# Soft mixture of experts after a causal attention and an MLP on one core: the slot weighting of three of four batches moved into the last MLP

## What is computed

```python
# 1 attention with a causal mask and a decay from the running sum of log f
scores = q @ k.T / 8 + (cum_i - cum_j)          # masked above the diagonal
x = softmax(scores) @ v                         # to (2304, 512)
# 2 MLP
h = x @ w_in                                    # (2304, 2048)
x = (h * sigmoid(1.702 * h)) @ w_out            # (2304, 512)
# 3 soft mixture of experts: 8 experts, 4 slots each = 32 slots
logits = x @ phi                                # (2304, 32)
d = exp(logits - logits.max(0)); d /= d.sum(0) + 1e-9      # over all tokens
slot_input = d.T @ x                            # (32, 512), 4 rows per expert
slot_out[e] = relu(slot_input[e] @ w1[e]) @ w2[e]          # 512 -> 1024 -> 512
c = exp(logits - logits.max(1)); c /= c.sum(1) + 1e-9      # over the slots
result = c @ slot_out                           # (2304, 512)
```

## Time and profile before

| | us |
|---|---|
| median of three runs | 764.37 (763.54 to 765.16) |
| the profiled execution, its own time | 765.94 |
| its span, first to last instruction | 764.2 |
| mean granted clock of TensorE | 0.983 of full |
| PE busy | 717.7 (94% of the span) |
| DVE / ACT / POOL busy | 444.7 / 437.0 / 399.3 |
| chain that ended last | PE 79%, DVE 10%, ACT 7%, issue 2% |

### The profile page before, as it was taken

How to read it: one execution, slowest core, us unless ns; L and a number is a source line. 1 busy time by engine, 2 the same in 40 slices (tenths; PEclk the granted TensorE clock), 3 DMA queues, 4 the chain that set the end, 5 groups by cost and what they waited for, 6 DMA issues and landing times.

```text
span 764.2 us, 15776 instructions
## 1 busy us (share of the span) xinstructions
PE 717.7 (94%) x6027; PEld 681.0 (89%) x6027; DVE 444.7 (58%) x1255; ACT 437.0 (57%) x1031; POOL 399.3 (52%) x439
## 2 busy tenths in 40 slices
PE   3999979999999999999999999999999999998993
PEld 3888879999999999999999989999999999995562
DVE  5898957676776646675656466766542332224323
ACT  4788866575757675666576665757554344311113
POOL 4355357474747764565657564848385476520000
PEclk9999989999999999999999999999999999998897
DMA  4433323332333333333331413332214454598976
GB/s 104 106 92 106 94 65 89 87 94 81 95 94 96 95 94 81 87 105 91 100 91 51 126 28 95 94 108 67 69 43 141 135 169 163 161 401 348 357 307 247
DMA packets 90362, 96.65 MB, mean 126 GB/s; under 512 B 61296, under 2 KB 61296, under 8 KB 88240
## 3 DMA queue, kind: packets, MB, share of 16 engines
q1 hardware_dynamic: 90288, 95.66, 40.6%
HBM read 90.84 MB, written 4.79 MB: 125 GB/s over the span
## 4 chain that ended last, share of the span: by engine, by line
PE 79%; DVE 10%; ACT 7%; issue 2%; DMA 0%; POOL 0%; SPq 0%; DVEq 0%; POOLq 0%
PE mb L1204 51%; PE yb L1057 6%; PE zb L1076 6%; PE xb L1103 5%; PE mb L1256 2%; DVE prob L838 2%; PE xb L1037 2%; ACT prob L689 2%; PE yb L1295 1%; ACT xh L713 1%; DVE ptl L844 1%; PE yb L1059 1%; DVE kl L806 1%; DVE qs L802 1%; ACT qs L681 1%
## 5 line engine op out<-in xcount | busy, mean ns | idle before, releaser
L1204 PE MATMUL mb<-xh,wih 128*128 128x288 f32 x512 | 159.1, 311 | 7.8 <-DVE xl L855 4.3
L1204 PE MATMUL mb<-gh,woh 128*128 128x288 f32 x512 | 156.5, 306 | 3.5 <-DVE x2t L932 3.5
L1204 PE MATMUL mb<-xl,wih 128*128 128x288 f32 x512 | 151.6, 296 | 0.0
L1204 PE MATMUL mb<-xh,wil 128*128 128x288 f32 x512 | 151.6, 296 | 0.0
L1204 PE MATMUL mb<-gl,woh 128*128 128x288 f32 x512 | 150.8, 294 | 0.0
L1204 PE MATMUL mb<-gh,wol 128*128 128x288 f32 x512 | 150.8, 294 | 0.0
L643 POOL TENSOR_TENSOR gl<-hid,gh 128x288 fp32r<-128x288 f32 x128 | 105.0, 825 | 74.9 <-ACT gh L730 73.3
L925 DVE SCALAR_TENSOR_TENSOR hid<-gate,mb 128x288 f32<-128x288 f32 x128 | 57.7, 451 | 116.0 <-ACT gate L736 114.9
L689 ACT ACTIVATE prob<-prob,m_row 64x576 f32<-64x576 f32 (+4 forms) x160 | 96.4, 604 | 35.3 <-DVE m_row L824 34.4
L660 POOL TENSOR_TENSOR wol<-stage,woh 128x512 fp32r<-128x512 f32 x64 | 82.9, 1295 | 62.0 <-ACT woh L675 62.0
L660 POOL TENSOR_TENSOR wil<-stage,wih 128x512 fp32r<-128x512 f32 x64 | 82.1, 1290 | 57.0 <-ACT wih L675 56.9
(11 more groups left out here) (196 smaller groups left out, 1471.1 us busy)
## 6 DMA issues: line engine op xcount, KB each, us to landing
stage<-in_moe_w_in SPq DMA_DIRECT2D x64, 256.0 KB, 3.0
stage<-in_moe_w_out SPq DMA_DIRECT2D x64, 256.0 KB, 2.6
ring_a<-in_moe_w SPq DMA_DIRECT2D x16, 1024.0 KB, 6.9
ring_b<-in_moe_w SPq DMA_DIRECT2D x14, 1024.0 KB, 11.8
cum_b<-cum_dram SPq DMA_DIRECT2D x32, 288.0 KB, 3.7
qk_in<-in_q SPq DMA_DIRECT2D x32, 144.0 KB, 3.0
qk_in<-in_k SPq DMA_DIRECT2D x32, 144.0 KB, 3.5
v_in<-in_v SPq DMA_DIRECT2D x32, 128.0 KB, 3.2
```

The costliest lines, as they stand in the source:

```text
L1204: ins = mm(bank[:, 0:HALF], a[:, t, P * (j % 4):P * (j % 4) + P], x[:, t, cols], start=(i == 0), stop=(i == 11))
```

## The change

Steps of kind `early` are put into the list of the last MLP. On the data of batches 0 to 2 (15 tiles) they make the maximum per slot, the weights `ew`, their exp, their sum (`all_sum`) and the 15 weighting products, kept unscaled in `acc`. Batch 3 is weighted after the last unit with its own maximum per row of its slot-major logits (`bmax`, `low_max`), without turning the logits first, by exp with a sum on ACT (`et`), a turn of the result (`ewt`), and 5 weighting products. `kept` rescales `acc`, and the factor between the row's maximum and that of all four column groups (`factor`), with the reciprocal of the sum, goes into the selecting matrix `sel_f`. The turned logits of batch 3, needed for c alone, are made after the experts' input. `post 1` turns the first two of four column tiles of tokens 256 to 575 before unit 63; `post 2` does the rest, with the slot logits of the first three of four tiles of the contraction ahead of the wait for unit 63's eviction. The ring has 11 places: `ring_x` becomes two, loaded in units 33 to 47; `ring_a` is loaded in quarters at each odd unit up to 31; matrices 0 to 5 are loaded inside the MLP. The constant products are 4, 2, 8 and 5 where they were 9, 3 and 14. The tile memory is laid out anew to fit. Two memsets of `mb` and `yb` (L970, L971) go. In the diff below the removed lines of the joint (L941 to L973, L1212 to L1246) and declarations are left out, and from the loads on twelve leading spaces of each line.

```diff
 LAST_POST = ((0, 1), (2, 3, 4))
+AHEAD = 2
...
-TURN_AT = 6
+TURN_AT = 7
 SOFTMAX_AT = (8, 9, 10, 11, 18, 19, 20, 21)
 SOFTMAX_EXP = 13
-BUSY = (9, 3, 14)
+BUSY = (4, 2, 8, 5)
+EARLY = 3 * QT
+EARLY_AT = {"maxima": 10, "turn_max": 12, "max": 13, "spread": 15, "weigh": 16, "exp": 17, "sums": 19,
+            "send0": 20, "send1": 21, "send2": 22, "send3": 23, "total": 24, "keep": 26}
+RING_X_AT = 33
...
+        if m == BATCH - 1:
+            steps += [(0, ("early", kind)) for kind in EARLY_AT if EARLY_AT[kind] == u]
...
-    return (held_steps(m) + mlp_steps(m, 0, U_MLP - 2) + [(0, ("post", 0))]
-            + mlp_steps(m, U_MLP - 2, U_MLP) + [(0, ("post", 1))])
+    return (held_steps(m) + mlp_steps(m, 0, U_MLP - 2) + [(0, ("post", 0))] + mlp_steps(m, U_MLP - 2, U_MLP - 1)
+            + [(0, ("post", 1))] + mlp_steps(m, U_MLP - 1, U_MLP) + [(0, ("post", 2))])
...
-        ring = ring_a + ring_b + [ring_x[:, :]]
+        ring = ring_a + ring_x + ring_b
...
-        if last and j == 2:
+        if last and u % 2 and u // 8 < len(ring_a):
             sp.wait_ge(x_lo, 4 * BATCH)
-            load_half_expert(u // 16, u % 16 // 8)
+            load_expert_part(u // 8, u // 2 % 4, 4)
+        at = u - RING_X_AT
+        if last and at >= 0 and at % 2 == 0 and at // 8 < len(ring_x):
+            sp.wait_ge(acc_made, 1)
+            load_expert_part(len(ring_a) + at // 8, at // 2 % 4, 4)
...
         sp.wait_ge(unit_done, m * U_MLP + U_MLP - 8)
-        load_expert(4)
-        load_expert(5)
+        load_expert(6)
+        load_expert(7)
...
-        load_expert(6)
+        load_expert(8)
...
+        load_expert(9)
+        load_expert(10)
...
+    elif st == ("early", "exp"):
+        act.wait_ge(ew_sub, 1)
+        nc.scalar.activation(ew[:, :, :], ew[:, :, :], ACT.Exp).then_inc(ew_exp, 1)
...
+    elif st == ("post", 1):
+        for i in LAST_POST[1]:
+            act.wait_ge(post_token, m * QT + i + 1)
+            nc.scalar.copy(x2last[0:QW[i], i, 0:P * AHEAD], last_tokens[i][0:QW[i], 0:P * AHEAD]
+                           ).then_inc(ahead_out, 1)
+    elif st == ("post", 2):
+        act.wait_ge(max_made, 2)
+        nc.scalar.activation(et[:, :], last_logits[:, 0:P + 64], ACT.Exp, bias=low_max[:, 1:2],
+                             accum_out=bsum[:, :]).then_inc(e_made, 1)
+        nc.scalar.activation(kept[:, :], low_max[:, 0:1], ACT.Exp, scale=-1.0, bias=low_max[:, 1:2]
+                             ).then_inc(kept_made, 1)
+        act.wait_ge(post_token, m * QT + QT + 2)
+        nc.scalar.copy(x2last[:, 2, P * AHEAD:MODEL], last_tokens[2][:, P * AHEAD:MODEL]).then_inc(token_out, 1)
...
-nc.scalar.activation(ew[:, :, :], ew[:, :, :], ACT.Exp).then_inc(t_act, 1)
+nc.scalar.copy(x2last[:, 3, P * AHEAD:MODEL], last_tokens[3][:, P * AHEAD:MODEL]).then_inc(token_out, 1)
+act.wait_ge(top_spread, 1)
+act.wait_ge(top_made, 1)
+nc.scalar.activation(factor[:, :], top_back[:, 0:1], ACT.Exp, bias=top[:, 0:1]).then_inc(factor_made, 1)
+nc.scalar.copy(lt[0:SLOTS, P:P + 64], last_logits[0:SLOTS, P:P + 64])
+nc.scalar.copy(lt[:, 0:P], last_logits[:, 0:P]).then_inc(lt_last, 1)
...
+        early(st[1])
+    elif st == ("post", 0):
+        nc.vector.memset(last_logits[32:64, P:P + 64], -3e38)
+        nc.vector.memset(last_logits[64:P, P:P + 64], -3e38).then_inc(edge_made, 1)
+    elif st == ("post", 2):
         dve.wait_ge(post_logits, m + 2)
-        keep_turned(last_logits)
-        dve.wait_ge(lt_turned, m + 1)
-        keep_logits(last_turn)
-        keep_maxima(m)
-        keep_values(m)
+        nc.vector.tensor_reduce(bmax[:, :], last_logits[:, 0:P + 64], AX_X, ALU.max).then_inc(max_raw, 1)
+        dve.wait_ge(max_raw, 1)
+        nc.vector.tensor_scalar(low_max[:, 1:2], bmax[:, :], -1.0, low_max[:, 0:1], ALU.mult, ALU.min
+                                ).then_inc(max_made, 1)
     elif st[0] == "unit":
         unit(b, m, st[1])
+def early(kind):
+    if kind == "maxima":
+        for i in range(4):
+            at = ident[32 * i:32 * i + 32, 32 * i:32 * i + 32]
+            nc.vector.tensor_copy(sel4[32 * i:32 * i + 32, :], at)
+            ins = nc.vector.tensor_copy(blk4[32 * i:32 * i + 32, :, :],
+                                        at.unsqueeze(1).broadcast_to([32, 4, SLOTS]))
+        ins.then_inc(sel_made, 1)
+        dve.wait_ge(l_kept, 2 * BATCH - 2)
+        nc.vector.tensor_reduce(gmax[:, :], gm[:, 0:BATCH - 1, :].rearrange("p b s -> p s b"), AX_X, ALU.max
+                                ).then_inc(gmax_made, 1)
+    elif kind == "max":
+        dve.wait_ge(gmax_turned, 1)
+        nc.vector.tensor_reduce(smax[:, :], top_row[0:SLOTS, 0:P], AX_X, ALU.max).then_inc(smax_made, 1)
+        dve.wait_ge(smax_made, 1)
+        nc.vector.tensor_scalar(dmax[:, :], ident[0:SLOTS, 0:SLOTS], smax[:, 0:1], None, ALU.mult
+                                ).then_inc(dmax_made, 1)
+    elif kind == "weigh":
+        dve.wait_ge(early_spread, 1)
+        nc.vector.tensor_tensor(ew[:, :, :], logits[:, :, :],
+                                top_back[:, 0:SLOTS].unsqueeze(1).broadcast_to([P, EARLY, SLOTS]),
+                                ALU.subtract).then_inc(ew_sub, 1)
+        nc.vector.tensor_scalar(low_max[:, 0:1], top_back[:, SLOTS:SLOTS + 1], -1.0, None, ALU.mult
+                                ).then_inc(max_made, 1)
+        nc.vector.memset(es4[:, 1:4, :], 0.0)
+    elif kind == "sums":
+        dve.wait_ge(ew_exp, 1)
+        nc.vector.tensor_reduce(es4[:, 0, :], ew[:, :, :].rearrange("p t s -> p s t"), AX_X, ALU.add
+                                ).then_inc(es_made, 1)
+    elif kind == "keep":
+        dve.wait_ge(early_den, 1)
+        nc.vector.tensor_copy(all_sum[:, 0:1], top_row[:, 0:1]).then_inc(sum_made, 1)
+        dve.wait_ge(early_sent, 1)
+        nc.vector.tensor_copy(acc[:, :], early_sent_ps).then_inc(acc_made, 1)
 def keep_turned(bank):
     nc.vector.tensor_copy(lt[0:SLOTS, P:P + 64], bank[0:SLOTS, P:P + 64])
...
+m = BATCH - 1
+dve.wait_ge(max_made, 2)
+nc.vector.tensor_scalar(top[:, :], low_max[:, 1:2], -1.0, None, ALU.mult).then_inc(top_made, 1)
+dve.wait_ge(post_token, m * QT + QT + 3)
+nc.vector.tensor_copy(x2last[0:64, 4, P * AHEAD:MODEL], last_tokens[4][0:64, P * AHEAD:MODEL]).then_inc(token_out, 1)
+dve.wait_ge(top_turned, 1)
+nc.vector.tensor_reduce(row_s[:, :], top_row[0:1, 0:P].rearrange("o (g s) -> o s g", g=4), AX_X, ALU.min
+                        ).then_inc(row_made, 1)
+dve.wait_ge(row_made, 1)
+nc.vector.tensor_copy(row[:, :, :], row_s[:, :].unsqueeze(1).broadcast_to([1, 4, SLOTS])).then_inc(row_made, 1)
+dve.wait_ge(e_turned, 1)
+nc.vector.tensor_copy(ewt[0:64, 4, :], last_turn[0:64, P:P + SLOTS])
+nc.vector.tensor_copy(ewt[:, 0:4, :], last_turn[:, 0:P].rearrange("p (i n) -> p i n", n=SLOTS)).then_inc(ewt_made, 1)
+dve.wait_ge(kept_made, 1)
+dve.wait_ge(sum_made, 1)
+nc.vector.tensor_scalar(all_sum[:, 1:2], all_sum[:, 0:1], kept[:, 0:1], bsum[:, 0:1], ALU.mult, ALU.add
+                        ).then_inc(sum_made, 1)
+dve.wait_ge(sum_made, 2)
+dve.wait_ge(factor_made, 1)
+nc.vector.tensor_tensor(part_sum[:, :], all_sum[:, 1:2], factor[:, :], ALU.mult).then_inc(den_in, 1)
+dve.wait_ge(den_made, 1)
+nc.vector.tensor_scalar(den[:, :], top_row[:, 0:1], EPS, None, ALU.add).then_inc(den_added, 1)
+dve.wait_ge(den_added, 1)
+nc.vector.reciprocal(rden[:, :], den[:, :]).then_inc(den_added, 1)
+dve.wait_ge(den_added, 2)
+nc.vector.tensor_scalar(sel_f[:, :], sel4[:, :], factor[:, 0:1], rden[:, 0:1], ALU.mult, ALU.mult
+                        ).then_inc(sel_scaled, 1)
+dve.wait_ge(sent, 1)
+dve.wait_ge(acc_made, 1)
+nc.vector.scalar_tensor_tensor(out=acc[:, :], in0=acc[:, :], scalar=kept[:, 0:1], in1=last_sent,
+                               op0=ALU.mult, op1=ALU.add).then_inc(acc_made, 1)
+dve.wait_ge(slots_summed, 1)
+nc.vector.tensor_copy(slot_t[:, :, :], slot_ps[:, 0:KM * SLOTS].rearrange("p (t s) -> p t s", t=KM)).then_inc(slot_made, 1)
...
+    elif st == ("post", 1):
+        pe.wait_ge(unit_out, m * U_MLP + U_MLP + 2 - 2)
+        for i in LAST_POST[1]:
+            turn_last(i, 0, AHEAD).then_inc(post_token, 1)
+    elif st == ("post", 2):
+        pe.wait_ge(unit_out, m * U_MLP + U_MLP + 2 - 1)
+        slot_logits(last_logits, LAST_POST[1], 0, KM - 1)
+        pe.wait_ge(unit_out, m * U_MLP + U_MLP + 2)
+        slot_logits(last_logits, LAST_POST[1], KM - 1, KM).then_inc(post_logits, 1)
+        pe.wait_ge(ahead_out, len(LAST_POST[1]))
+        for i in LAST_POST[1]:
+            turn_last(i, AHEAD, KM).then_inc(post_token, 1)
...
+    if kind == "turn_max":
+        pe.wait_ge(gmax_made, 1)
+        pe.wait_ge(logits_out, 1 + 2 * (BATCH - 1))
+        pe.wait_ge(token_out, 1 + (BATCH - 1) * QT)
+        tr(top_row[0:SLOTS, 0:P], gmax[:, :], ident[:, :]).then_inc(gmax_turned, 1)
+    elif kind == "spread":
+        pe.wait_ge(dmax_made, 1)
+        pe.wait_ge(sel_made, 1)
+        mm(top_back[:, 0:SLOTS], ones[0:SLOTS, :], dmax[:, :], start=True, stop=True)
```

(54 more changed lines are left out.)

269 lines of the change are left out of this document (138 added, 131 removed).

## The result

The changed kernel takes 767.07 us (median of 20 runs, 765.74 to 769.13); the kernel before, run beside it, 765.13 us (20 runs, 761.71 to 768.09). The ratio is **1.0028, 95% interval 1.0016 to 1.0040**: a little slower, where 758.4 us, a gain of 6.0, was forecast.

The account below looks back on a forecast made before the run. PE was taken to bound the last MLP, and a chain of waits between engines the joint. Terms +5.1 (MLP), -7.3 (joint) and -3.8 (clock) sum to -6.0 us, from 764.37 to 758.4 us; range 756.2 to 760.

Parts of the forecast that it names:

- The clock: First expert: PE's clock stays at 2.4 GHz, so `up(0)`, `up(1)` and the work between save 3.8 us; bounds 0 and 4.1.
- the joint: Last unit's eviction to first expert product: 16.0 us shrinks to 8.7, so -7.3 us; bounds 7.6 and 11.5.
- after it all is as before: From `up(2)` on nothing changes: 29.2 us to the last `down`, 21.1 to the end, set by the stores.
- Added to the MLP: Last MLP, on PE's path: the work moved in lengthens it by 5.1 us; bounds 4.3 and 6.2.
- the sends: Last MLP: fifteen weighting products in four groups at 0.90 us each cost PE 3.6 us.
- SP's queue: Last MLP: ring matrices loaded in quarters among the stage loads cost PE 0, bound 0.3 us.
- the cover of 1.4 us: Last MLP: a quarter's last low half of weights is ready at 606.86, its units start at 608.3, so lateness is absorbed.
- Rival 3: Units 8 to 48 of the MLP: stage loads become late, losing 7.5 us over six sets; about 766; chance 0.05.
- the summing products: Joint, ahead of the experts' input: 2.04 us at a clock of 0.68 becomes 1.4 us at full clock.
- Rival 1: Joint and first expert: the clock falls all the same, a whole fall costing 3.8 us; 760.3 to 762.2; chance 0.15.
- Loads: Expert matrices: with two more ring places they finish by 726 to 730, ahead of their last user at 737.
- rival 2: Joint: it does not shrink as worked out, because of engine handovers; at 11.5 us it gives 761.2; chance 0.08.

Follow-up runs that it names:

- paced: Changed kernel, tiles left off 256-byte multiples, with loads of matrices 0 to 5 as halves, one per four units, instead of quarters: 765.55 us, 1.0013.
- edge_early: Changed kernel with the two memsets of `last_logits` moved from `post 0` to the early step `keep`: 767.57 us, 1.0033.
- before_busy: Kernel before with ten more constant products, eight behind the sum of the weights and two behind the summing products: 763.52 us, 1.0000.
- best0: Changed kernel realigned, memsets early, loads in halves, the four sends in one step, no constant products in the tail: 761.82 us, 0.9966.
- best: Changed kernel realigned, memsets early, loads in halves, the four sends in one step, constants 4, 2, 3, 3: 761.91 us, 0.9968.
- best8: Changed kernel realigned, memsets early, loads in halves, the four sends in one step, constants kept at 4, 2, 8, 5: 763.32 us, 0.9988.
- the aligned kernel: Changed kernel with two one-column tiles made one, putting the tiles behind them back on multiples of 256 bytes: 764.42 us, 1.0006.

## Why the prediction was wrong

Most of it is the MLP: the work moved into it costs 8.0 to 10.3 us, not 5.1. The clock gives some 1.3 us, not 3.8, a change of layout that the prediction didn't count costs 1.7 to 3.3, and the joint gives 6.4, not 7.3.

**The layout had no term.** The front tells that the tile memory is laid out anew, and the prediction goes past it. It is worth 1.7 or 3.3 us by the two ratios. It could have been read: the address of a tile is a sum of the sizes ahead of it, and the page of the Trainium skill that I cited for the order of queues (DMA: Bandwidth & Descriptors) states the rule of 256 bytes. Nor did "after it all is as before" hold: stores cost 1.1 us more, and the experts 0.6 in the changed kernel's trace.

**Added to the MLP: +5.1 was +8.0, and up to +10.3.** Term by term, on the chains of before and paced, where no load is in the way (102.17 us from 591.30 to T0 against 94.49 from 592.11, +7.68):
- the sends: 3.6 was 4.75, of it 3.99 the products and 0.76 the four units behind them;
- the sum, the turned maximum and `spread`: 0.33, 0.13 and 0.3 were 0.12, 0.11 and 0.53. The six turns: 0.8 was 0.66;
- draining, a bound of mine and no term, was some 0.4 more in the units behind the small products (60 products in 8.11 us, where 7.95 would be their share of 660 in 87.44 before);
- `edge_made`: 0.95, in no part of the text. I had counted waits of the early steps and not the new one in `post 0`, whose memsets stand behind an eviction on DVE. The cause is shown by edge_early.

These make 7.5 of the 7.7. The rest of the changed kernel's is *SP's queue*: 0 with a bound of 0.3 was 0.4 in one trace and some 2.6 in the other. The step that failed is the cover of 1.4 us. Three of the four landings in the two chains (3.61, 4.07, 5.51 and 5.96 us) are within the 5.65 that the prediction allowed, and they cost PE time all the same: it set against that cover what *one* load is late by at the last low half, and saw neither ACT's order, in which a load holds up the next tanh, nor the series, in which one late load sends out the next one late. The prediction also argued from the Trainium skill (DMA: Bandwidth & Descriptors, Queues, rings and completion order) that nothing issued behind a load could delay it. The page states the ring order of descriptors, and beside it that a later one may finish its write before an earlier one; the rest was my inference, and no run here tests it alone. Rival 3 had its place right, and its price three times too high.

**The joint: -7.3 was -6.4.** Up to the fifth product the forecast's 5.4 was 5.74, the turns of the logits 0.40 for 0.26, the eight constants 1.04, and the summing products 1.83, not 1.4. I had scaled 2.04 us at a clock of 0.68 by the clock alone, and that step was wrong in kind: at a full clock the same eight products take 2.07 us in before_busy and 2.04 in best0, against 2.09 in the kernel before. That the constants outlast DVE's addition and set the joint was right, and is a fault of the change (best: 9.08, best0: 8.87).

**The clock: -3.8 was about -1.3.** The changed kernel's own trace bears the forecast out, a clock of 1.00 from T0 to the mixing, and would have deceived me. Over the traces with its joint, `up(0)` to `up(2)` is 7.37, 9.13, 7.37, 8.65, 9.02 and 9.18, mean 8.45; before it is 11.17, 9.62 and 8.59, mean 9.8. Six and three traces that scatter by 1.8 and 2.6 us give this difference only roughly. Rival 1 (0.15) should have had most of the chance, and its counterpart too, that the kernel before doesn't always lose 3.8. The reason I gave against it, no gap over 0.4 us, is refuted by best8, whose PE stands idle 0.01 us in the joint and whose clock falls. The Trainium skill (TensorE: Matmul & The Clock Gate, Part 1) lets the clock fall after idleness; best8, with 0.01 us of it in 9.70, doesn't agree as to this fall. What decides it in one execution and not in the next is open.

**Loads and rival 2** were right: in the changed kernel's trace no matrix is waited for, and the joint is no longer than its bounds.

**The sum.** For the aligned kernel +8.4 - 6.4 - 1.3 = +0.7 us; measured 1.0006, 0.5 us, to within 1.2, so that the two meet so closely is luck. With the tiles off it is 1.7 or 3.3 more: 1.0028 and 1.0049. And 0.8 us of the miss is only that the kernel before has 765.13 in the runs beside the result, not 764.37.

**The range.** Its lower end, 756.2, is the sum of the bounds; its upper end, 760, isn't. The upper bounds of the prediction's own terms are 6.2 and twice 0.3 in the MLP, 11.5 for the joint and 0 for the clock: 6.8 - 4.5 = +2.3, which is 766.7.

So where did 16 us of joint go? Down to 9.5 as meant, but the work taken out of it costs PE more where it stands now than it cost in the joint, at first sight idle time: 6.4 gained, 6.6 (the 7.5 above less the wait of 0.95) paid on an engine that has nothing to spare. The change pays only by what is put right around it.

## What to carry to other kernels

Work moved from a latency-bound joint into a PE-bound stage costs its PE time in full, and more if it comes in pieces: keep small products in one block, and take every new wait with what stands ahead of its setter on that engine. After any change of layout look at the addresses of the tiles that transfers touch: 32 bytes past a multiple of 256 cost this kernel 0.2 to 0.4%. Before giving credit for a clock that rises, look at several traces of the kernel before, and leave the constant products out once to see whether they do anything.
